# Second FFN of an attention kernel: seven block products for eight in its first matrix, and the second matrix summed on VectorE

## What is computed

```python
def _moe_ref(x, w_a, w_b, w_out):          # 384 -> 1536 -> 384
    a = x @ w_a
    b = x @ w_b
    return (a * b @ w_out)

def _moe2_ref(x, domain_probs, w1, w2):    # N=3072, D=384, E=4, F=1024
    p = domain_probs / (domain_probs.sum(-1, keepdims=True) + 1e-09)
    for e in range(E):
        h = np.maximum(x @ w1[e], 0.0)
        out += p[:, e:e + 1] * (h @ w2[e])
    return out
```

## Time and profile before

| | us |
|---|---|
| median of three runs | 1409.36 (1407.99 to 1411.0) |
| profiled execution, its own time | 1409.11 |
| span of that execution | 1407.3 |
| TensorE busy | 1386.9 (99%) |
| VectorE busy | 480.2 (34%) |
| ScalarE busy | 391.8 (28%) |
| GpSimd busy | 271.7 (19%) |

### The profile page before, as it was taken

How to read it: one execution, slowest core, us unless ns; L and a number is a source line. 1 busy time by engine, 2 the same in 40 slices (tenths; PEclk the granted TensorE clock), 3 DMA queues, 4 the chain that set the end, 5 groups by cost and what they waited for, 6 DMA issues and landing times.

```text
span 1407.3 us, 19724 instructions
## 1 busy us (share of the span) xinstructions
PE 1386.9 (99%) x7897; PEld 1287.3 (91%) x7897; DVE 480.2 (34%) x932; ACT 391.8 (28%) x739; POOL 271.7 (19%) x215
## 2 busy tenths in 40 slices
PE   7899999999999999999999999999999999999999
PEld 6799999999999999989999999999999999999998
DVE  7786555545532222212222222222222222222222
ACT  4444433434322222232111311212311112211111
POOL 4442221212110100141111411111511113211110
PEclk6799999999999999999999999999999999999999
DMA  6552222222200000020000200000200001000001
GB/s 146 156 136 64 64 48 59 64 62 47 50 14 12 12 1 1 1 70 23 0 1 1 70 21 1 0 1 11 80 1 0 1 0 35 12 23 23 24 23 45
DMA packets 43693, 49.34 MB, mean 35 GB/s; under 512 B 4688, under 2 KB 42064, under 8 KB 43600
## 3 DMA queue, kind: packets, MB, share of 16 engines
q1 hardware_dynamic: 43600, 48.04, 13.0%
HBM read 38.58 MB, written 4.72 MB: 31 GB/s over the span
## 4 chain that ended last, share of the span: by engine, by line
PE 96%; issue 0%; DVE 0%; ACT 0%; DMA 0%; SPq 0%; DVEq 0%
PE bank L1035 21%; PE bank L1036 20%; PE bank L1037 20%; PE bank L1166 10%; PE bank L1165 10%; PE bank L1164 9%; PE bank L1000 2%; PE bank L1030 2%; PE bank L1009 1%; PE bank L1023 1%; PE bank L985 1%; DMA xt<-ystage 0%; ACT xs_hi L564 0%; DVE ostage L961 0%; DVE wab_lo L816 0%
## 5 line engine op out<-in xcount | busy, mean ns | idle before, releaser
L968 DVE SCALAR_TENSOR_TENSOR h_lo<-bank,h_hi 128x512 fp32r<-128x512 f32 x192 | 132.7, 691 | 599.8 <-ACT h_hi L648 599.8
L648 ACT ACTIVATE h_hi<-bank 128x512 fp32r<-128x512 f32 x192 | 114.8, 598 | 627.4 <-PE bank L1037 627.4
L1166 PE MATMUL bank<-slot_hi,h_lo 128*128 128x384 f32 x768 | 258.5, 337 | 0.0
L1164 PE MATMUL bank<-slot_hi,h_hi 128*128 128x384 f32 x768 | 258.2, 336 | 0.0
L1165 PE MATMUL bank<-slot_lo,h_hi 128*128 128x384 f32 x768 | 258.1, 336 | 0.0
L1035 PE MATMUL bank<-xs_hi,slot_hi 128*128 128x512 f32 x576 | 225.4, 391 | 1.8 <-issue 1.8
L1036 PE MATMUL bank<-xs_hi,slot_lo 128*128 128x512 f32 x576 | 226.2, 393 | 0.0
L1037 PE MATMUL bank<-xs_lo,slot_hi 128*128 128x512 f32 x576 | 226.0, 392 | 0.0
L1035 PE MATMUL bank<-xs_hi,wab_hi 128*128 128x384 f32 x576 | 200.2, 348 | 6.7 <-ACT xs_hi L564 6.7
L1036 PE MATMUL bank<-xs_hi,wab_lo 128*128 128x384 f32 x576 | 194.7, 338 | 0.0
L1037 PE MATMUL bank<-xs_lo,wab_hi 128*128 128x384 f32 x576 | 194.3, 337 | 0.0
(11 more groups left out here) (87 smaller groups left out, 1501.5 us busy)
## 6 DMA issues: line engine op xcount, KB each, us to landing
unit<-fkq SPq DMA_DIRECT2D x62, 216.0 KB, 4.2
raw<-w SPq DMA_DIRECT2D x64, 192.0 KB, 2.6
v_in<-v_chunks SPq DMA_DIRECT2D x32, 144.0 KB, 3.9
out<-ostage SPq DMA_DIRECT2D x24, 192.0 KB, 1.9
xt<-ystage SPq DMA_DIRECT2D x48, 72.0 KB, 2.2
raw<-wa SPq DMA_DIRECT2D x6, 384.0 KB, 3.8
raw<-wb SPq DMA_DIRECT2D x6, 384.0 KB, 3.4
raw<-wo SPq DMA_DIRECT2D x6, 384.0 KB, 3.6
```

Source lines behind the costliest of these rows:

```text
L648: eng.activation(h_hi[:, j % 2, :], ps_up[j % 4][:, :], ACT.Relu).then_inc(s_hhi, 1)
L968: eng.scalar_tensor_tensor(out=h_lo[:, j % 2, :], in0=ps_up[j % 4][:, :], scalar=0.0, in1=h_hi[:, j % 2, :].bitcast(f32), op0=ALU.max, op1 ...
L1164: eng.matmul(o, hh, w_hi, start=(f == 0), stop=False)
L1166: mm = eng.matmul(o, hl, w_hi, start=False, stop=(f == FT2 - 1))
```

## The change

Only the second FFN and what feeds it are altered.

- **Loops.** Blocks of 768 tokens are outside (NP = 4), then experts, then groups of 256 hidden features (FP = 4): GP = 16 groups a block, G = 64 in all.
- **First matrix.** A group is a product of w1 (384 x 256) and x (384 x 768 tokens). Two of its three k tiles and both of its feature and token halves form 2x2 blocks, multiplied by Winograd's form of Strassen's scheme: seven block products, of which several use sums of blocks (S1 to S4 of w1, T1 to T4 of x). The third k tile is multiplied plainly, four products. Each of the eleven is three matmuls of 384 columns (`product`). A product that several of the four results share stays in its bank, and is copied to SBUF (`copy`, ScalarE) before the bank is added to further; the copy and the later bank are then summed by `add` (VectorE). `h2_round` and `h2_rest` split the result from SBUF.
- **Sums.** `up_sums` (VectorE) forms S1 to S4 of each group in `w_s` from `raw`; `x2_sums` forms T1 to T4 once a token block. They are split like all other operands.
- **Second matrix.** `down_2` sums over the two feature tiles of a group in PSUM; six token tiles of 128 then go to `weigh` after every group, 384 weighings in place of 96, added to `acc`, which takes the place of x in `xt`. The tiles lie in the banks that the up products of the same parity use.
- **Weights.** Each group loads 384 KB of w1 and 384 KB of w2 again for every token block (`load_w1`, `load_w2`), into rings of three.
- **Moved into the first FFN's slots**: sums and splits of the first x block, w1 of group 0, the sums of group 1.

The general path is adapted alike and is left out here.

```diff
+    NP = NB1 // 2
+    FP = FT2 // 2
+    GP = E * FP
+    G = NP * GP
+    TT = 2 * TB1 // 128
...
+    B11, B21, B22, B31, B32, T1, T2, T3, T4 = range(9)
+    X_ORDER = (B11, B21, B22, B31, B32, T1, T3, T2, T4)
+    X_FROM = {B11: (0, 0), B21: (1, 0), B22: (1, 1), B31: (2, 0), B32: (2, 1)}
+    NX = len(X_ORDER)
+    A11, A21, A12, A22, A13, A23, S1, S2, S3, S4 = range(10)
+    C11, C21, C12, C22 = range(4)
+    H_ORDER = (C11, C12, C22, C21)
+    C_STEP = {C11: 4, C12: 6, C22: 7, C21: 8}
+    C_COPY = {C11: 1, C12: 3, C22: 2, C21: 4}
+    STEPS = 8
...
+        def wu_free(eng, g):
+            if g == 0:
                 eng.wait_ge(s_upb, FT1 * (NB1 - 1))
-            elif g == 1:
-                eng.wait_ge(s_upb, N1)
+            elif g < RING2:
+                eng.wait_ge(s_down, N1)
             else:
-                eng.wait_ge(s_up, (g - 1) * FT2)
...
+        def acc(b, t):
+            return xt.rearrange("p b k s -> p b (k s)")[:, b, t * DM:(t + 1) * DM]
+        def tile_bank(g, t):
+            return UP_SETS[g % 2][(2, 3, 0, 1, 2, 3)[t]][:, 0:DM]
...
+            def load_w1(g):
+                if g == 0:
+                    eng.wait_ge(s_whi, R1)
+                    eng.wait_ge(s_wlo, R1)
+                else:
+                    eng.wait_ge(s_uhi, 2 * g - 1)
+                    eng.wait_ge(s_ulo, 2 * g - 1)
+                    eng.wait_ge(s_ws, 4 * g)
+                _, e, f = group(g)
+                eng.dma_start(raw[:, 0, :].rearrange("p (k f) -> p k f", k=KT),
+                              w1[e, :, f * 256:(f + 1) * 256].rearrange("(k p) f -> p k f", p=128)).then_inc(s_w1, 16)
+            def load_w2(g):
+                if g == 0:
+                    eng.wait_ge(s_whi, R1)
+                    eng.wait_ge(s_wlo, R1)
+                else:
+                    eng.wait_ge(s_dhi, g)
+                    eng.wait_ge(s_dlo, g)
+                _, e, f = group(g)
+                eng.dma_start(raw[:, 1, :].rearrange("p (i n) -> p i n", i=2),
+                              w2[e, f * 256:(f + 1) * 256, :].rearrange("(i p) n -> p i n", p=128)).then_inc(s_w2, 16)
...
+            for g in range(G):
+                if g + 2 < G:
+                    load_w1(g + 2)
+                if g + 1 < G:
+                    load_w2(g + 1)
+                if g % GP == 0 and g > 0:
+                    store_out(g // GP - 1)
+            store_out(NP - 1)
+            eng.wait_ge(s_out, 16 * NT)
...
+            def up_round(g):
+                wu_free(eng, g)
+                eng.wait_ge(s_w1, 16 * (g + 1))
+                eng.activation(wu_hi[g % RING2][:, 0:6, :], raw[:, 0, :].rearrange("p (a f) -> p a f", a=6), ACT.Copy)\
+                   .then_inc(s_uhi, 1)
+            def up_sums_round(g):
+                eng.wait_ge(s_ws, 4 * (g + 1))
+                eng.activation(wu_hi[g % RING2][:, 6:10, :], w_s[:, :, :], ACT.Copy).then_inc(s_uhi, 1)
+            def down_round(g):
+                wd_free(eng, g)
+                eng.wait_ge(s_w2, 16 * (g + 1))
+                eng.activation(wd_hi[g % RING2][:, :, :], raw[:, 1, :].rearrange("p (i n) -> p i n", i=2), ACT.Copy)\
+                   .then_inc(s_dhi, 1)
+            def copy(g, n):
+                o, role, step = ((C11, 0, 1), (C22, 1, 2), (C12, 0, 3), (C21, 0, 5))[n]
+                eng.wait_ge(s_step, STEPS * g + step)
+                if g >= 1:
+                    eng.wait_ge(s_h2lo, 4 * (g - 1) + H_ORDER.index(o) + 1)
+                eng.activation(h2[:, o, :], UP_SETS[g % 2][role][:, 0:TB1], ACT.Copy).then_inc(s_copy, 1)
+            def h2_round(g, n):
+                eng.wait_ge(s_add, 4 * g + n + 1)
+                if g >= 2:
+                    eng.wait_ge(s_tile, TT * (g - 1))
+                o = H_ORDER[n]
+                eng.activation(h2_hi[:, g % 2, o, :], h2[:, o, :], ACT.Relu).then_inc(s_h2hi, 1)
 
...
+            up_round(1)
+            for g in range(G):
+                copy(g, 0)
+                copy(g, 1)
+                if g == 0:
+                    up_sums_round(1)
+                copy(g, 2)
+                copy(g, 3)
+                if g == 0:
                     y_out(NB1 - 1)
-                for r in late_pieces(j):
-                    split_hi(r)
-                if f == 2 and g + 1 < E * NB:
-                    x2_hi(g + 1)
+                for n in range(4):
+                    h2_round(g, n)
+                if g == 0:
+                    down_round(0)
+                if g + 2 < G:
+                    up_round(g + 2)
+                if g + 1 < G:
+                    down_round(g + 1)
+                if g + 2 < G:
+                    up_sums_round(g + 2)
+                if (x := x2_next(g)) is not None:
+                    x2_round(*x)
...
+            def up_rest(g):
+                eng.wait_ge(s_uhi, 2 * g + 1)
+                eng.tensor_tensor(wu_lo[g % RING2][:, 0:6, :], raw[:, 0, :].rearrange("p (a f) -> p a f", a=6),
+                                  wu_hi[g % RING2][:, 0:6, :].bitcast(f32), ALU.subtract).then_inc(s_ulo, 1)
+            def up_sums_rest(g):
+                eng.wait_ge(s_uhi, 2 * g + 2)
+                eng.tensor_tensor(wu_lo[g % RING2][:, 6:10, :], w_s[:, :, :], wu_hi[g % RING2][:, 6:10, :].bitcast(f32),
+                                  ALU.subtract).then_inc(s_ulo, 1)
+            def down_rest(g):
+                eng.wait_ge(s_dhi, g + 1)
+                eng.tensor_tensor(wd_lo[g % RING2][:, :, :], raw[:, 1, :].rearrange("p (i n) -> p i n", i=2),
+                                  wd_hi[g % RING2][:, :, :].bitcast(f32), ALU.subtract).then_inc(s_dlo, 1)
 
...
+            up_rest(1)
+            up_sums_rest(1)
+            down_rest(0)
+            for g in range(G):
+                if g + 2 < G:
+                    up_rest(g + 2)
+                if g + 1 < G:
+                    down_rest(g + 1)
+                if g + 2 < G:
+                    up_sums_rest(g + 2)
+                if (x := x2_next(g)) is not None:
+                    x2_rest(*x)
...
+            def up_sums(g):
+                eng.wait_ge(s_w1, 16 * (g + 1))
+                if g == 0:
+                    eng.wait_ge(s_y, NU)
+                    for n in range(2):
+                        eng.wait_ge(s_x[n], x_all[n])
+                else:
+                    eng.wait_ge(s_uhi, 2 * g)
+                    eng.wait_ge(s_ulo, 2 * g)
+                a11, a21, a12, a22 = (raw[:, 0, i * 128:(i + 1) * 128] for i in (A11, A21, A12, A22))
+                s1, s2, s3, s4 = (w_s[:, i, :] for i in range(4))
+                eng.tensor_tensor(s1, a21, a22, ALU.add).then_inc(s_ws, 1)
+                eng.tensor_tensor(s3, a11, a21, ALU.subtract).then_inc(s_ws, 1)
+                eng.wait_ge(s_ws, 4 * g + 1)
+                eng.tensor_tensor(s2, s1, a11, ALU.subtract).then_inc(s_ws, 1)
+                eng.wait_ge(s_ws, 4 * g + 3)
+                eng.tensor_tensor(s4, a12, s2, ALU.subtract).then_inc(s_ws, 1)
 
...
+            def add(g, n):
+                o = H_ORDER[n]
+                role = {C11: 2, C12: 1, C22: 0, C21: 3}[o]
+                eng.wait_ge(s_step, STEPS * g + C_STEP[o])
+                eng.wait_ge(s_copy, 4 * g + C_COPY[o])
+                eng.tensor_tensor(h2[:, o, :], h2[:, o, :], UP_SETS[g % 2][role][:, 0:TB1], ALU.add).then_inc(s_add, 1)
...
+            def weigh(g, t):
+                b, e, f = group(g)
+                w = pn[:, b * TT + t, e:e + 1]
+                d = tile_bank(g, t)
+                eng.wait_ge(s_tile, TT * g + t + 1)
+                if e == 0 and f == 0:
+                    eng.tensor_scalar(acc(b, t), d, w, None, ALU.mult).then_inc(s_acc, 1)
+                else:
+                    eng.wait_ge(s_acc, TT * (g - 1) + t + 1)
+                    eng.scalar_tensor_tensor(out=acc(b, t), in0=d, scalar=w, in1=acc(b, t),
+                                             op0=ALU.mult, op1=ALU.add).then_inc(s_acc, 1)
+            y_out_1(NB1 - 1)
             eng.wait_ge(s_pn, 4)
-            for j in range(N2):
-                i = N1 + j
-                eng.wait_ge(s_hhi, i + 1)
-                eng.scalar_tensor_tensor(out=h_lo[:, j % 2, :], in0=ps_up[j % 4][:, :], scalar=0.0,
-                                         in1=h_hi[:, j % 2, :].bitcast(f32), op0=ALU.max,
-                                         op1=ALU.subtract).then_inc(s_hlo, 1)
-                if j == 0:
-                    y_out_1(NB1 - 1)
-                elif j % FT2 == 0:
-                    weigh(j // FT2 - 1)
-            weigh(E * NB - 1)
+            for g in range(G):
+                add(g, 0)
+                add(g, 1)
+                h2_rest(g, 0)
+                add(g, 2)
+                h2_rest(g, 1)
+                add(g, 3)
+                h2_rest(g, 2)
+                h2_rest(g, 3)
+                for t in range(TT):
+                    if g >= 1:
+                        weigh(g - 1, t)
+                    if t == 1 and g + 2 < G:
```

(135 more changed lines are left out.)

303 lines of the change are left out of this document (154 added, 149 removed).

## The result

The changed kernel takes 1473.11 us (median of four runs, 1472.11 to 1473.43) against 1408.67 for the kernel before: ratio 1.0454, 95% interval 1.0436 to 1.0472. It is 64 us slower, with fewer columns to multiply.

The account below looks back on a forecast made before the run. TensorE was taken to bound the kernel, busy for 1386.9 of 1407.3 us. Sum: 1409.1 - 31 (matmuls) + 82 (stall) + 11 (entry) + 3 (stores) = 1474 us; range 1440 to 1520, own range 1448 to 1500.

Parts of the forecast that it names:

- Matmuls, -31: Second FFN: fewer matmul columns on TensorE save 0.49 us a group over 64 groups, 31 us.
- The stall, +82: Each up's start: TensorE waits 1.35 us for a weighing behind sums held by GpSimd, 61 times, 82 us.
- The reading of the rows at 62 and 67 us: Old trace: GpSimd got in between back-to-back VectorE operations; a subtract took 1.88 us instead of 0.55.
- Entry, +11: Entry into the second FFN: one TensorE stall of about 9 us plus some 2 us of slower clock.
- Stores, +3: Three token block ends: six stores ahead of the next w1 load cost 1 us each, bounds 0 and 10.
- the copies: ScalarE's four copies inside up: taken as 0, bounds 0 and 0.7 us a group.
- (a): VectorE's sums: it keeps its turn or misses GpSimd, so TensorE doesn't stall; 1392 us, chance 0.15.
- (b): Inside up: the four copies are late too, 22 to 45 us more, 1496 to 1519; chance 0.12.
- the margin of 0.05 us: Inside up: about 0.05 us by which a copy fits ahead of the next weight load, thinnest in the plan.
- (c): TensorE's clock gives way to the pauses, 1.5 us for each of 61, giving 1565 us; chance 0.05.

Follow-up runs that it names:

- e2: Changed kernel with ScalarE and GpSimd taking w2 of the next group behind the sums of w1, VectorE's order unchanged: 1386.64 us.
- e8: Changed kernel's loops with the first matrix multiplied plainly, twelve block products a group, no sums, copies or adds: 1409.98 us.
- e1: Changed kernel with VectorE forming the sums of w1 at the start of the iteration, ahead of the adds: 1389.23 us.
- e4: Changed kernel with ScalarE's entry order altered: w2 of group 0 rounded early, group 1's copies ahead of the weight rounding of groups 1 and 2: 1467.73 us.
- e9: Changed kernel with GpSimd's w2 remainder in two halves, one ahead of the remainder of the sums, one behind it: 1422.67 us.
- e3: Changed kernel with ScalarE rounding the sums of w1 one step later, between the second and third copy of the next group: 1471.89 us.
- e6: Changed kernel with three more 384-column matmuls in each down, at the start of its last token tile: 1474.31 us.
- e7: e1 with three more 384-column matmuls in each down, at the start of its last token tile: 1422.45 us.
- e5: e2 with ScalarE's entry reordered: w2 of group 0 early, group 1's copies first, weights of groups 2 and 1 after group 1's results: 1382.84 us.

## Why the prediction was right

Forecast 1474, measured 1473.1. The mechanism is the one that was forecast; that the sum is right to 1 us is in part luck, since the terms' errors cancel. By its steps:

- **Matmuls, -31.** The period that is left when nothing waits is 12.00 us (e2) against 12.50: 0.50 x 64 = 32. Right to 1 us.
- **The stall, +82.** e2 lies 86.5 us below the changed kernel, 1.42 us for each of 61 groups, against 1.35 forecast. The order of events came as worked out: sum 1 to the end of the first remainder, second remainder in between, sums 2 to 4 behind it. In the iteration around 1004, with t = 0 at 1001.03, sum 4 ended at 6.92 (worked out: 6.94), weigh 2 at 7.45 (7.47), and TensorE started at 7.59 (7.62). What the term lacked is the restart: the first matmul after the wait takes 0.26 us to the next (1008.62 to 1008.88) instead of 0.17. The load of the second's weights goes out only at 1008.70, 0.18 us before it, not ahead of the first's start. The reading of the rows at 62 and 67 us, that GpSimd gets its turn between two operations of VectorE that stand back to back, carried the sign; half a dose of it left 36.0 of the 86.5 us.
- **Entry, +11.** From the changed kernel's own rows (first matmul at 602.01, last one's start 866.2 us later, 768 us of it the periods of 12.00, 86.5 the stall) 11.7 are left. TensorE stood for 8.5 us, forecast 9; the slow clock cost 3.2, forecast 2, since it fell twice: behind the pause, as forecast, and already at 602.66. e8 has neither.
- **Stores, +3: wrong.** SyncE issued six stores in 6.52 us at 829.26, the next w1 went out at 835.90, and the gaps of TensorE at 833.99 and 847.40 are the common ones. Cost 0. The load went out 2.5 us late (13.4 us after 819.99 would be 833.4) and, landing in 3.6, was still there 2 us before its user on ScalarE at 841.45; in e2, with a period of 12.0, TensorE shows no gap either. The cost exists where the load has less room: 2.3 us in e1.
- In its place the second FFN began 1.8 us earlier than before (602.01 against 603.77). In the nine profiles of kernels with the seven for eight that start lies between 600.8 and 602.6, in the two without (before and e8) at 603.8 and 604.3; no cause was looked for.

So 1409.1 - 32 + 86.5 + 11.7 - 1.8 = 1473.5. The forecast's own range of 1448 to 1500 is narrower than its bounds make it: added up they give 1438 to 1507, without the copies. Of the rivals, (a) is what e1 and e2 are, and its price of 1392 fits their 1389 and 1387. (b), the copies: in e2 TensorE has no gap in 360 us, so four copies of 1.01 us fit into 1.22 with the weight load as well; the margin of 0.05 us held. (c), the clock: it stayed at 1.00 from 640 us on through a pause of 1.4 us in every 13.4. The evidence that was put against (c) is weaker than it looked, though. The pause of some 2 us ahead of the second FFN left 1.00 behind it in the kernel before, in e4, e8 and e9, and was followed by 0.83 over 600 to 610 in the changed kernel, e1, e2, e3, e6 and e7, and by ten slow matmuls in e5. What decides between the two isn't shown here.

## What to carry to other kernels

Before a change puts work on an idle-looking engine, write down, in order, what stands beside each new operation on an engine that it was seen to take turns with: four sums worth 1 us cost 86 us here because they came up across two queued GpSimd operations, and the order of two lines was worth more than the whole gain in matmuls. When a bound engine shows a gap, put work into the gap: if it is free, look along the chain that sets the period, not at the busy shares. The releaser that the profile names was the last event before the start here, and not the one waited for; check it against what the code waits for.
